# Experts of a top-1 mixture layer take 256 tokens at a time instead of 128, with the first weights stationary, and the slot table's one-hots come from wide operations

## What is computed

```python
for b in range(B):
    prev_e = -1
    for s in range(S):
        fresh_e = int(np.argmax(logits[b, s]))
        if s == 0 or local_gate[b, s] < 0.5:
            e = fresh_e
        else:
            e = prev_e if prev_e >= 0 else fresh_e
        prev_e = e
        ...
        h = np.maximum(x[b, s] @ w1[e], 0.0)     # 512 -> 1024
        out[b, s] = p[e] * (h @ w2[e])           # 1024 -> 512
```

## Time and profile before

| | us |
|---|---|
| three runs, median | 496.53 (495.94 to 497.08) |
| the profiled execution, its own time | 496.07 |
| its span, first to last instruction | 494.3 |
| PE busy | 458.2 (93%) |
| DVE busy | 260.5 (53%) |
| ACT busy | 210.9 (43%) |
| POOL busy | 92.7 (19%) |

### The profile page before, as it was taken

The page is one execution under the profiler, slowest core; times in us unless marked ns, Lnnn a source line. Parts: engine busy times, 40 slices in busy tenths (PEclk is TensorE's granted clock), DMA queues, the critical chain, the costliest instruction groups (busy, mean ns, idle before and its releaser), DMA issues.

```text
span 494.3 us, 7689 instructions
## 1 busy us (share of the span) xinstructions
PE 458.2 (93%) x2635; PEld 390.7 (79%) x2636; DVE 260.5 (53%) x421; ACT 210.9 (43%) x337; POOL 92.7 (19%) x137
## 2 busy tenths in 40 slices
PE   5399999589999999999999998399999999999997
PEld 5388888478887877887878786289889889889985
DVE  2268696529192828373746465496454534525401
ACT  0114333036372737282828283386444633615400
POOL 2215872532222222222122221100000000000000
PEclk9599999899999999999999999799999999999999
DMA  5899994027475655556585710610010000010001
GB/s 108 257 406 374 350 346 184 2 66 249 177 228 198 225 201 198 207 206 218 181 328 171 253 42 23 214 62 1 21 45 0 21 21 21 0 42 21 0 23 42
DMA packets 28552, 70.86 MB, mean 143 GB/s; under 512 B 3248, under 2 KB 4272, under 8 KB 28528
## 3 DMA queue, kind: packets, MB, share of 16 engines
q1 hardware_dynamic: 22992, 57.94, 33.7%
q0 software_dynamic: 2800, 9.18, 5.5%
q10 hardware_dynamic: 2736, 3.43, 2.1%
HBM read 59.01 MB, written 11.01 MB: 142 GB/s over the span
## 4 chain that ended last, share of the span: by engine, by line
PE 80%; DVE 8%; DMA 3%; issue 3%; SPq 2%; POOL 1%; DVEq 1%; ACT 0%; POOLq 0%; ACTq 0%
PE bank L1023 21%; PE bank L1025 20%; PE bank L1024 20%; DVE wl L789 5%; PE bank L953 3%; PE bank L929 3%; PE bank L942 2%; PE bank L963 2%; PE bank L1047 2%; PE bank L971 2%; DMA qk_sb<-in_qk_dram 2%; PE bank L1033 2%; POOL slot_row L405 1%; PE bank L917 1%; PE bank L978 1%
## 5 line engine op out<-in xcount | busy, mean ns | idle before, releaser
L789 DVE TENSOR_TENSOR wl<-raw,wh 128x1024 fp32r<-128x1024 f32 x64 | 74.6, 1218 | 0.0
L508 ACT ACTIVATE wh<-raw 128x1024 fp32r<-128x1024 f32 x64 | 64.0, 1052 | 0.0
L783 DVE TENSOR_TENSOR hl<-bank,hh 128x512 fp32r<-128x512 f32 x32 | 22.1, 690 | 64.1 <-ACT hh L504 64.1
L1023 PE MATMUL bank<-wh,hh 128*128 128x512 f32 x128 | 52.7, 412 | 2.6 <-DVE hl L783 1.6
L1023 PE MATMUL bank<-wh,xh 128*128 128x512 f32 x128 | 51.4, 402 | 1.7 <-DVE xl L779 1.7
L1025 PE MATMUL bank<-wh,hl 128*128 128x512 f32 x128 | 50.1, 391 | 0.0
L1025 PE MATMUL bank<-wh,xl 128*128 128x512 f32 x128 | 50.0, 391 | 0.0
L1024 PE MATMUL bank<-wl,hh 128*128 128x512 f32 x128 | 50.0, 390 | 0.0
L1024 PE MATMUL bank<-wl,xh 128*128 128x512 f32 x128 | 49.8, 389 | 0.0
L499 ACT ACTIVATE h_sb<-bank 128x512 f32<-128x512 f32 x32 | 19.1, 596 | 64.6 <-PE bank L1025 64.6
L1023 PE MATMUL bank<-xkh,wh 128*128 128x384 f32 x128 | 43.1, 336 | 1.1 <-DVE xkl L855 1.1
(11 more groups left out here) (159 smaller groups left out, 892.7 us busy)
## 6 DMA issues: line engine op xcount, KB each, us to landing
raw<-in_w_dram SPq DMA_DIRECT2D x64, 512.0 KB, 8.4
qk_sb<-in_qk_dram SPq DMA_DIRECT2D x12, 512.0 KB, 7.8
kv_sb<-in_kv_dram SPq DMA_DIRECT2D x12, 512.0 KB, 6.7
x_dram<-keep ACTq DMA_DIRECT2D x12, 256.0 KB, 5.9
keep<-y_dram SPq DMA_DIRECT2D x12, 256.0 KB, 5.1
out_dram<-o_sb SPq DMA_DIRECT2D x12, 256.0 KB, 2.0
raw<-in_w_k_dram SPq DMA_DIRECT2D x4, 512.0 KB
raw<-in_w_v_dram SPq DMA_DIRECT2D x4, 512.0 KB
```

The lines of the kernel that those rows point to most:

```text
L508: act.activation(parts[1 - p][0][:, c, :], raw[:, c, :], ACT.Copy).then_inc(s["part_h"], 1)
L783: dve.tensor_tensor(hl[:, 4 * g:4 * g + 4, :], by(psT[g][:, :], 4), hh[:, 4 * g:4 * g + 4, :].bitcast(F32), ALU.subtract).then_inc(s["hl_d ...
L789: dve.tensor_tensor(parts[1 - p][1][:, c, :], raw[:, c, :], parts[1 - p][0][:, c, :].bitcast(F32), ALU.subtract).then_inc(s["part_l"], 1)
L1023: pe.matmul(ps, lhsT=a_high, rhs=b_high, start=start, stop=False)
```

## The change

**Units of 256 tokens.** An expert takes units of `PAIR` = 256 tokens, at least one. With the token counts above there are 8 units in place of 16 tiles. Two gathers fill `x_tok[0]` and `x_tok[1]`, and `xh`, `xl`, `hh`, `hl` are twice as wide.

**First weights stationary.** In `h_products` a 128x128 piece of w1 is stationary and 256 columns of x stream past, so h comes out features by tokens. The h transposes and the separate relu copy are gone: ACT reads the PSUM bank once with a relu (`h_high`), DVE once (`h_low`). h of a unit takes 96 matmuls of 256 columns (before, in two tiles: 48 of 512 columns). y still takes 48 matmuls of 512 columns for two tiles.

**Where the weights are split.** ACT and DVE split chunks 0 to 5 of the next expert ahead of the unit, and the last `CH_LATE` = 2 chunks behind it. PE waits for the first six before the h products, and for all eight before the y products.

**The slot table.** DVE makes `col_hit` and `slot_row` in two operations each (576 and 768 columns), POOL multiplies to get `slot_col` in two operations of 576 columns. The plan has more steps on DVE, since POOL now walks over units with a table `unit_col`.

```diff
-    MIN_TILES = 2
+    PAIR = 2 * P
+    CH_LATE = 2
+    PARTS = FIRST + CH_LATE
 # SP: a chunk of raw is free
-                sp.wait_ge(s["part_l"], FIRST + r * CH + c + 1)
+                sp.wait_ge(s["part_l"], PARTS + r * CH + c + 1)
 # POOL: slot table
-            for n in range(NT):
-                pool.tensor_scalar(slot_row[:, n, :], iota_row[:, :], row[:, n:n + 1], None, ALU.is_equal).then_inc(s["slot_row_done"], 1)
+            for b in range(B):
+                pool.wait_ge(s["col_hit_done"], b + 1)
+                pool.tensor_tensor(slot_col[:, b * NC:(b + 1) * NC, :], col_hit[:, b * NC:(b + 1) * NC, :], per_token(value, b),
+                                   ALU.mult).then_inc(s["slot_col_done"], 1)
 # ACT
-            def relu_h(i, g):
-                act.wait_ge(s["h_ps"], i * 2 + g + 1)
-                act.activation(h_sb[:, g * D:(g + 1) * D], bank[g][:, :], ACT.Relu).then_inc(s["h_done"], 1)
-            def h_high(i, g):
-                act.wait_ge(s["hT_ps"], i * 2 + g + 1)
-                act.activation(hh[:, 4 * g:4 * g + 4, :], by(psT[g][:, :], 4), ACT.Copy).then_inc(s["hh_done"], 1)
+            def h_high(u, f):
+                act.wait_ge(s["h_ps"], u * 4 + f + 1)
+                act.activation(hh[:, 2 * f:2 * f + 2, :], by(psH[f][:, :], 2), ACT.Relu).then_inc(s["hh_done"], 1)
-                    tile(lo, e, p)
+                    act.wait_ge(s["raw_in"], (e + 1) * (16 * CH))
+                    act.sem_inc(s["act_passed"], 1)
+                    for c in range(CH - CH_LATE):
+                        weights_high(p, c)
                     if j < UNROLL - 1:
                         hi_next = plan_ahead(act, e)
-                    with act.Fori(lo + 1, hi) as i:
-                        tile(i)
+                    with act.Fori(lo, hi) as u:
+                        unit(u)
+                    for c in range(CH - CH_LATE, CH):
+                        weights_high(p, c)
 # DVE: slot table
-            for n in range(NT):
-                dve.tensor_scalar(slot_col[:, n, :], iota_row[:, 0:COLS], col[:, n:n + 1], value[:, n:n + 1],
-                                  ALU.is_equal, ALU.mult).then_inc(s["slot_col_done"], 1)
+            for b in range(B):
+                dve.tensor_tensor(col_hit[:, b * NC:(b + 1) * NC, :], iota_row[:, 0:COLS].unsqueeze(1).to_broadcast([P, NC, COLS]),
+                                  col[:, b * NC:(b + 1) * NC].unsqueeze(2).to_broadcast([P, NC, COLS]), ALU.is_equal).then_inc(s["col_hit_done"], 1)
+                dve.tensor_tensor(slot_row[:, b * NC:(b + 1) * NC, :], iota_row[:, :].unsqueeze(1).to_broadcast([P, NC, P]),
+                                  row[:, b * NC:(b + 1) * NC].unsqueeze(2).to_broadcast([P, NC, P]), ALU.is_equal).then_inc(s["slot_row_done"], 1)
 # DVE: a unit
+            def unit(u):
+                for f in range(4):
+                    h_low(u, f)
+                y_copy(u, 0)
+                for a in range(2):
+                    x_low(u + 1, a)
+                y_copy(u, 1)
+                    for c in range(CH - CH_LATE):
+                        weights_low(e, p, c)
+                    with dve.Fori(lo, hi) as u:
+                        unit(u)
+                    for c in range(CH - CH_LATE, CH):
+                        weights_low(e, p, c)
 # PE
+            def h_products(p, f):
+                for i in range(2):
+                    cols = slice((2 * f + i) * P, (2 * f + i + 1) * P)
+                    for c in range(KD):
+                        mm = three_products(psH[f][:, i * PAIR:(i + 1) * PAIR], [w[:, c, cols] for w in w1p[p]],
+                                            [x[:, c, :] for x in (xh, xl)], start=(c == 0), stop=(c == KD - 1))
+                mm.then_inc(s["h_ps"], 1)
+            def unit(u, e, p):
+                pe.wait_ge(s["xl_done"], u * 2 + 2)
                 for f in range(4):
+                    h_products(p, f)
+                pe.wait_ge(s["part_l"], e * CH + PARTS)
+                pe.wait_ge(s["y_done"], u * 2 + FIRST)
+                y_products(u, p, 0)
+                x_unit_transposes(u + 1)
+                y_products(u, p, 1)
```

More of the change, by code:

```diff
@@ L176, in mixer_kernel @@
         value = sb("value", [P, NT])
[L177 to L180, removed]
+        x_slots = sb("x_slots", [P, 2], U32)
+        y_slots = sb("y_slots", [P, 2], U32)
         cnti = sb("cnti", [1, E], I32)
@@ L208, in mixer_kernel @@
         o_out = [sem(f"s_o_out{i}") for i in range(3)]
+        x_in = [sem(f"s_x_in{i}") for i in range(2)]
+        y_out = [sem(f"s_y_out{i}") for i in range(2)]
         y_in = [sem(f"s_y_in{i}") for i in range(NT)]
@@ L219, in plan_of, with all_units @@
         def plan_of(eng, e):
-            lo = eng.value_load(plan[0:1, bass.ds(e, 1)], min_val=0, max_val=NTILES_MAX)
-            hi = eng.value_load(plan[0:1, bass.ds(e + 1, 1)], min_val=MIN_TILES, max_val=NTILES_MAX)
+            lo = eng.value_load(plan[0:1, bass.ds(e, 1)], min_val=0, max_val=UNITS_MAX - 1)
+            hi = eng.value_load(plan[0:1, bass.ds(e + 1, 1)], min_val=1, max_val=UNITS_MAX)
             return lo, hi
         def plan_ahead(eng, e):
-            return eng.value_load(plan[0:1, bass.ds(e + 2, 1)], min_val=MIN_TILES, max_val=NTILES_MAX)
-        def column(c, e):
-            return nc.s_assert_within(c, e * NT, e * NT + NT - 1, skip_runtime_bounds_check_because="an expert has no more tiles than all tokens fill")
+            return eng.value_load(plan[0:1, bass.ds(e + 2, 1)], min_val=1, max_val=UNITS_MAX)
+        def all_units(eng):
+            return eng.value_load(plan[0:1, E:E + 1], min_val=E, max_val=UNITS_MAX)
         def yT_at(n):
@@ L392, in _ @@
             decayed_k(1)
-            pool.dma_start(x_dram[N:N + P, :], zrows[:, :]).then_inc(s["pad_out"], 16)
+            for a in range(2):
+                pool.dma_start(x_dram[N + a * P // 2:N + (a + 1) * P // 2, :], zrows[0:P // 2, :]).then_inc(y_out[a], 16)
             for t in range(2, NT):
@@ L417, in scatter @@
[L417 to L447, removed]
+            def per_token(x, b):
+                return x[:, b * NC:(b + 1) * NC].unsqueeze(2).to_broadcast([P, NC, COLS])
@@ new lines, in _ @@
+            pool.wait_ge(s["x_stored"], 16 * NT)
+            for x in y_out:
+                pool.wait_ge(x, 16)
+            pool.wait_ge(s["slots_done"], 1)
+            fetch(slots)
+            pool.wait_ge(s["plan_done"], 1)
+            total = all_units(pool)
+            with pool.Fori(0, total) as u:
+                c = pool.value_load(unit_col[0:1, bass.ds(u, 1)], min_val=0, max_val=COLS - 2)
+                next_c = pool.value_load(unit_col[0:1, bass.ds(u + 1, 1)], min_val=0, max_val=COLS - 2)
+                pool.wait_ge(s["x_ps_done"], u * 2 + 2)
+                pool.tensor_copy(x_slots[:, :], slots[:, bass.ds(next_c, 2)]).then_inc(s["x_slots_done"], 1)
+                pool.wait_ge(s["x_slots_done"], u + 1)
+                pool.sem_inc(s["pool_passed"], 1)
+                fetch(x_slots)
+                for a in range(2):
+                    pool.wait_ge(s["y_done"], u * 2 + FIRST + a + 1)
+                    pool.tensor_copy(y_slots[:, a:a + 1], slots[:, bass.ds(c + a, 1)]).then_inc(s["y_slots_done"], 1)
+                    pool.wait_ge(s["y_slots_done"], u * 2 + a + 1)
+                    pool.wait_ge(y_out[1 - a], u * 16 + a * 16 + 16)
+                    pool.sem_inc(s["pool_passed"], 1)
+                    pool.indirect_dma_start(out=y_dram[:, :], out_offset=bass.IndirectOffsetOnAxis(ap=y_slots[:, a:a + 1], axis=0),
+                                            in_=y_sb[a], in_offset=None).then_inc(y_out[a], 16)
@@ L449, in _ @@
+            for a in range(2):
+                pool.wait_ge(x_in[a], total * 16 + 16)
         @block.scalar
@@ L506, in weights_high @@
             def weights_high(p, c):
                 act.activation(parts[1 - p][0][:, c, :], raw[:, c, :], ACT.Copy).then_inc(s["part_h"], 1)
[L510 to L527, removed]
+            def unit(u):
+                for f in range(4):
+                    h_high(u, f)
+                for a in range(2):
+                    x_high(u + 1, a)
@@ L529, in _ @@
             act.wait_ge(s["exp_done"], 1)
+            act.wait_ge(s["x_stored"], 16 * NT)
+            for a in range(2):
+                x_high(0, a)
             act.wait_ge(s["plan_done"], 1)
-            act.wait_ge(s["mx_ps"], 1)
-            act.activation(xh, by(psX[:, :], KD), ACT.Copy).then_inc(s["xh_done"], 1)
             with act.Fori(0, E // UNROLL) as ep:
@@ L1025, in three_products @@
                 return pe.matmul(ps, lhsT=a_low, rhs=b_high, start=False, stop=stop)
-            def x_tile_transposes(n):
-                pe.wait_ge(s["x_in"], n * 16 + 16)
-                if not (isinstance(n, int) and n == 0):
-                    pe.wait_ge(s["xl_done"], n)
-                for a in range(KD):
```

(8 more changed lines are left out.)

200 lines of the change are left out of this document (95 added, 105 removed).

## The result

The changed kernel takes 534.22 us (533.48 to 534.92, 4 runs) against 496.63 (495.94 to 497.08): a ratio of 1.0758, 95% interval 1.0742 to 1.0774. It is 38 us slower. The forecast was 512, between 503 and 524.

The account below looks back on a forecast made before the run. PE was taken to bound the expert stage, busy 25.27 of 25.6 us. From 496.07: +10.9 weights, -0.8 slot table, +0.75 end, +4.5 clock gave 511.4; the median lies 0.46 higher, so 512, range 503 to 524.

Parts of the forecast that it names:

- What bounds the kernel, and what PE gains: Expert stage: PE is the bound; without h transposes PE alone needs 23.5 us per expert, 1.9 less than now.
- The rival with loads standing ahead of their matmuls: h products: unhidden weight loads make h 23 us, an expert 35, total 573; its whole rival group had chance 0.05.
- What the weights cost: Expert stage: PE waits 3.7 us for late weights; seven experts take 27.2 us against 25.37, stage sum +10.9.
- I take T + 6.6: Late chunks land, with ACT's wake-up, 6.6 us after T, when PE starts an expert's h products; bounds 5.9 and 8.45.
- the lone chunk: Weight load in the earlier trace: issued at 78.09, moved by 80.7 at 400 GB/s, 2.6 us; basis for the landing estimate.
- a least landing time of 5.2: Weight loads: least chunk landing time in the trace, used as upper bound, putting the landing at T + 8.45.
- The clock: PE's waits ahead of y products: three of seven lose the 2.4 GHz clock, 1.5 us each, +4.5 in sum.
- a sign of being wrong: Stated check on PE's seven waits: the forecast is wrong if the clock falls in all or in none.
- T + 11.6: Expert stage: moment when PE is through with h, 11.6 us after it starts the expert's h products.
- My second rival: Expert stage: slower landing, 525 us, or clock lost in every wait, 518; both 531; chance 0.17.
- The slot table: Start: `slots` at about 95.3, table gain taken as 1.9 us, less 1.08 for a second gather, net -0.8.
- The end: After the last y copy: low splits slow a POOL copy ahead of the last scatter, +0.75 us.

Follow-up runs that it names:

- experiment 2: Changed kernel, but the two late chunks land on their own semaphore, so ACT waits ahead of the unit for six chunks and the last y copy: 482.34 us, ratio 0.9729.
- Experiments 1: Changed kernel with no late chunks: all eight are split ahead of the unit, after ACT waits for the last y copy; 486.11 us, ratio 0.9806.
- experiment 4: Changed kernel with GpSimd's second scatter and next two gathers held until ACT has passed its wait for raw weights: 532.65 us, ratio 1.0757.
- Experiment 7: Changed kernel with one late chunk in place of two (CH_LATE = 1): 525.55 us, ratio 1.0598.
- Experiment 3: Changed kernel with 40 identity transposes on PE between the h and y products of each unit: 528.53 us, ratio 1.0658.
- experiment 5: Kernel before the change with only the wide slot-table operations added: 495.12 us against 496.24, ratio 0.9976.
- experiment 6: Kernel with six-chunk waits and a separate semaphore for late chunks, plus 16 identity transposes behind the first x transposes: 482.09 us, ratio 0.9715.
- experiments 3 and 8: The 8: changed kernel with both GpSimd's transfers held until the raw weights are in and 40 identity transposes in each wait; 526.6 us, ratio 1.0642.

## Why the prediction was right or wrong

**What bounds the kernel, and what PE gains: right.** The h transposes are gone, a 256-column matmul takes 0.120, and without the wait an expert takes 23.3 us (experiment 2) where the forecast had 23.5. The rival with loads standing ahead of their matmuls is out: a load of full height is on record for 0.195 us, 256 columns cost 0.108 by the slope of 0.054 for 128, and the step is 0.120, so the loads were overlapped. The rival's rule was the Trainium skill's sentence (TensorE: Matmul & The Clock Gate, Part 3) that a load overlaps only when it goes to other rows; the trace disagrees. The same section also names the background weight buffer as a second case in which a load is pulled ahead, and the overlap in the trace fits that case, though no run here shows the buffer itself.

**What the weights cost: the mechanism right, the size wrong.** Experiments 1 and 2 show that the loss is ACT's wait for the two chunks that an expert frees only at its end. The term that failed is the landing, "I take T + 6.6". It was 8.28 on average, 1.7 more in each of seven experts: 12 us. I had let both chunks move at 400 GB/s back to back, 1.3 us each; experiment 4 has about 2 us for each. The row had said as much: the traffic of the lone chunk in the earlier trace rows runs from 79.1 to 80.9, 1.8 us, since it starts and ends below 400. Experiment 7 has a chunk in ACT's hands 3.6 us after its issue, and a second adds about 2. The row that I put aside as a bound, a least landing time of 5.2, was nearer than the one lone chunk on which I built.

**The clock: the size wrong.** "I count three waits: +4.5." The clock fell in all seven, which the forecast had named as a sign of being wrong. The true waits, made longer by the landing, were 5.1 to 5.8 us. But that is not why the count failed: in experiment 7 the waits, counted in the same way from T + 11.6, were 3.8 to 4.0 in six experts and 4.9 in one, hardly more than the forecast's 3.7, and the clock fell in all seven too. The price was low as well: each y part took 13.8 in place of 11.9, where I had 1.5 for a lost clock. That is 13.2 us in all, 8.7 more than counted. Experiment 3 shows that it is the clock. (In the row from which I took the longer delay, the clock fell at 312.4, 4.6 us after PE stopped, not at 312.6.) My second rival held just these two together, the landing and the clock, at 531, with a chance of 0.17, and my range ended below it.

**The slot table: right in its time partly by luck, wrong in what follows.** `slots` came at 95.65 (forecast 95.3), 2.05 us earlier, but 0.7 of this was there before the table began: `row` starts at 89.34 in this execution and at 90.04 in the one before. The table itself gained 1.35 where I took 1.9, and experiment 5 shows its gain by itself, 1.2 us. PE began the first h product no earlier. The second gather was counted; not counted was the time after it: 1.1 us from the end of x's low part to the first matmul, where the kernel before has 0.17, put down to "issue". Since the change PE runs through one more load from `plan` and the entry of the unit loop ahead of its first product, which both stood behind the first tile; that they fill the gap is likely and not shown. And in this execution the clock fell after the pause, in the first expert, about 1.3 us (24.8 against 23.5); it did not in four others (experiment 6). The forecast of -0.8 for the start became 0.

**The end: right**, +0.8 for +0.75.

With the four corrections, 11.8 + 8.7 + 1.3 + 0.8, the sum of 511.4 becomes 534.0, against 534.27 for the profiled execution.

**Still open:** why experiment 3 delays ACT's start by 0.6 us, what holds PE ahead of the fifth expert in experiments 3 and 8, whether holding GpSimd's transfers gives anything once the clock is kept, and why the pause at the start loses the clock in some executions only. None of these touches the cause.

## What to carry to other kernels

When a buffer is freed piece by piece and refilled, the wait on the consumer should name only the pieces that it takes next: one wait for all eight chunks, where six were needed, turned a gain of 13 us into a loss of 38. If the broad wait also guarded something else, here the weights still in use, that needs a wait of its own. Before moving work behind the end of a stage, follow what it frees: here the moved splits released the loads, and everything that waited for those loads moved with them. And a new wait on PE of some microseconds is to be priced twice, once for itself and once for the clock that it loses.

## What the runs showed of the hardware

Two 512 KB loads issued 1.1 us apart on one queue, with the DMA engines otherwise idle, moved one behind the other, about 2 us each, at up to 410 GB/s within a block (experiment 4). A chunk with no other chunk beside it, only the scatter of 256 KB, was in use 3.6 us after its issue (experiment 7).

Waits of PE of 3.7 to 4.7 us, by the idle time of the profile, lost the 2.4 GHz clock in seven of seven experts (experiment 7), and so did waits of 4.9 to 5.6 us (the changed kernel). Forty transposes of the identity in these waits kept it in all fourteen of experiments 3 and 8, where at most 1.8 us of waiting was left.

A pause of 2.4 us at the start was followed by a fall to 1.2 GHz in three profiled executions and not in four, with the same program there. In the changed kernel the fall came when PE already worked again, 1.4 us into the first h products (fell at 106.1, PE from 104.71).
